# Windowed attention and two expert layers: queries, keys and values laid out as the products read them, value product turned round

## The chip, the cores and the metric

One core of one Trainium2 chip. The metric is the time on the device in microseconds, lower is better; the median of the runs shown is 935.2 us.

## The reference

Three layers stand behind each other, all in float32. First an attention of 4 batches x 8 heads x 768 positions x 64 numbers: each chunk of 32 queries sees 8 memory rows and a window of keys from 16 before the chunk to 8 after it, 64 columns in all.

```python
for c in range(nc):
    q_c = q[:, :, c_start:c_end]
    k_full = np.concatenate([mem_k, k[:, :, l_start:r_end]], axis=2)
    v_full = np.concatenate([mem_v, v[:, :, l_start:r_end]], axis=2)
    scores = scale * np.matmul(q_c, k_full.transpose(0, 1, 3, 2))
    a = np.exp(scores - np.max(scores, axis=-1, keepdims=True))
    a = a / (np.sum(a, axis=-1, keepdims=True) + 1e-09)
    out[:, :, c_start:c_end] = np.matmul(a, v_full)
```

Then `h = x @ w_in`, `g = h * cos(h)`, `g @ w_out` over 3072 rows (512 to 2048 to 512), and then eight experts (512 to 1024 to 512, relu), to which a router sends the rows whose skip score is positive, each with its gate.

## The kernel before, in words

A tile is 128 positions of one batch with all 8 heads; there are 24. Three tiles make a block of 384 rows; there are eight blocks, 0 to 7. PE does the products, ACT and DVE empty the accumulators, SP issues the loads, POOL fills constants and stores gates. The order on each engine is written out by hand and fixed; semaphores tie them.

**Middle layer.** For each of 16 rounds f of a block PE does `up(f)` (L758: 12 matmuls with 384 columns into one of two banks h_ps) and `down(f - 2)` (L774: 9 matmuls with 512 columns into three banks y_ps). Weights and rows are split in a high and a low float32r part, three matmuls per product. ACT takes h_ps out twice (L953, L954), makes the high part of g (L963) and the cosine as a sine (L977); DVE makes the fraction (L1190, L1192), g (L1185) and its low part (L1196). In round 1 ACT also takes the three y banks of the block before (L985, after the sine).

**Sites.** Between these products lie 32 sites a block: site 2f stands on PE behind `up(f)`, site 2f + 1 behind `down`. On ACT site 2f comes after h_ps is taken out, on DVE after g, and site 2f + 1 at the end of the round. ATTENTION (L39) puts the steps for the tiles of the next block on sites that start at 0, 10 and 20. ROUTER (L44) puts the router of the block before on others: x1 (transposes of the output rows, L737) at 4, 7 and 24, logits (L747) at 5, 8 and 25. On one site, steps run in the order of their names. PROLOGUE (L48) does the three tiles of block 0 ahead of everything; block 0 has no router, but splits weights (`in_high`, `in_low`, `out_high`, `out_low`) at the ends of its rounds. Block 7 has no attention.

**One tile of attention before.** SP loads 128 query rows, 4 windows of key rows, and 8 pieces of value windows (L410 to L447), in a batch's first tile also 12 pieces of memory rows; a row of a head is 64 numbers, 256 bytes. PE turns q (L667) and both halves of k (L676) with 4 transposes each, DVE copies q out (L1078), ACT k (L921). `scores` (L690) is 32 small products, 64 instructions: 64 rows of the array, 32 weight columns, 64 moving columns; the output row group is the chunk, and the two row halves of the array are the two heads of a pair, one half after the other. DVE finds the maximum and subtracts it (L1092, L1097), ACT takes the exponential (L926), DVE sums and forms the reciprocal (L1102 to L1106). PE turns the probabilities (L700), ACT copies them (L930), and `values` (L718) is again 32 products with 32 weight columns (probabilities) and 64 moving ones (values), into two banks, queries on partitions. DVE multiplies by the reciprocal (L1113), PE turns the result (L727), and ACT and DVE write its high and low part (L936, L1119), as `up` reads it. All transposes in blocks share one bank, `turn`; a semaphore counts its uses (L64).

Behind the blocks come a sort of the rows by expert and up to 20 slots of 256 rows through an expert each (L859).

Of the kernel before, what the change touches and what calls it, by code (L numbers as in the profile page):

```python
# [25 lines left out]
ALU = mybir.AluOpType  # L26
# [3 lines left out]
P = 128  # L30
CHUNK, LEFT, RIGHT = 32, 16, 8
# [16 lines left out]
PROLOGUE = [("q", 0), ("k0", 0), ("k1", 0), ("scores", 0), ("exp", 0), ("sum", 0), ("probs", 0), ("values", 0),  # L48
            ("q", 1), ("k0", 1), ("k1", 1), ("x", 0), ("w_in", 0), ("scores", 1), ("exp", 1), ("q", 2),
            ("k0", 2), ("k1", 2), ("sum", 1), ("probs", 1), ("w_in", 1), ("values", 1), ("scores", 2), ("x", 1),  # L50
            ("exp", 2), ("sum", 2), ("probs", 2), ("w_in", 2), ("values", 2), ("x", 2)]
SPLIT_FIRST = 3
T_STEPS = ("q", "k0", "k1", "probs", "x", "x1", "logits")
# [17 lines left out]
def program(nc, q, k, v, mem_k, mem_v, w_in, w_out, w_skip, w_gate, w1, w2, out, x_mid):  # L71
    NB, NH, S, HD = q.shape
    NMEM = mem_k.shape[2]
# [24 lines left out]
    with ctx:  # L98
# [37 lines left out]
        q_sb = sb("q_sb", [P, D])  # L136
        k_sb = sb("k_sb", [P, 2, D])
        v_sb = sb("v_sb", [P, CPT, HP * HD])
        qT = sb("qT", [P, HP, P])
        kT = sb("kT", [P, 2, HP, P])  # L140
        probs = sb("probs", [P, HP, 2, WIN])
        probsT = sb("probsT", [P, HP, P])
        x_sb = sb("x_sb", [P, HP, 2, HD])
# [18 lines left out]
        def pre(name, shape):  # L162
            size = 4 * shape[1] * shape[2] * shape[3]
            t = sb(name, shape, offset=at_pre[0])
            at_pre[0] += size
            return t

        q_pre = pre("q_pre", [P, 2, 1, D])
        k_pre = pre("k_pre", [P, 2, 2, D])
# [73 lines left out]
        first_full = {step: sem(f"first_full_{step}") for step in ("q", "k0", "k1", "probs", "x")}  # L243
        first_free = {step: sem(f"first_free_{step}") for step in ("q", "k0", "k1", "probs", "x")}
        pre_qk_ld = [sem(f"pre_qk_ld{n}") for n in range(2)]
        pre_v_ld = [sem(f"pre_v_ld{n}") for n in range(2)]
        memory_done = sem("memory_done")
# [6 lines left out]
        rsum_done = sem("rsum_done")  # L254
        v_full = sem("v_full")
        v_free = sem("v_free")
# [73 lines left out]
        first_bank = {"q": y_ps[:, 0, :], "k0": y_ps[:, 1, :], "k1": y_ps[:, 2, :], "probs": h_ps[:, 0, :], "x": h_ps[:, 1, :]}  # L330


# [6 lines left out]
        def bank(B, step):  # L339
            return first_bank[step] if is_first(B) else turn[:, 0, :]  # L340

        def filled(B, step):
            return first_full[step] if is_first(B) else t_full

        def freed(B, step):
            return first_free[step] if is_first(B) else t_free

        def wait_filled(eng, B, step, j):

            if is_first(B):  # L350
                eng.wait_ge(first_full[step], j + 1)
            else:
                eng.wait_ge(t_full, use(B, step, j) + 1)

        def wait_filled_before(eng, B, step, j):

            if is_first(B):
                wait(eng, first_full[step], j)
            elif j:
                eng.wait_ge(t_full, use(B, step, j - 1) + 1)  # L360
            else:
                wait_filled(eng, B - 1, step, BT - 1)

        def wait_freed(eng, B, step, j):

            if is_first(B):
                eng.wait_ge(first_free[step], j + 1)
            else:
                eng.wait_ge(t_free, use(B, step, j) + 1)

        def tile_of(B, j):

            return BT * (B + 1) + j

# [30 lines left out]
        def _(sp):  # L405
            def heads(array, b, par, lo, hi):

                picked = slice(0, NH) if par is None else slice(par, NH, 2)
                return array[bass.ds(b, 1), picked, lo:hi, :].rearrange("b h p d -> p (b h) d")

            def load_q(to, b, t, ld):
                sp.dma_start(to.rearrange("p (h d) -> p h d", d=HD), heads(q, b, None, t * P, (t + 1) * P)).then_inc(ld, 16)

            def load_k(to, b, t, ld):
                for c in range(CPT):
                    first = t * P + c * CHUNK - LEFT
                    lo, hi = max(first, 0), min(first + CTX, S)
                    r0 = (c % 2) * WIN + NMEM + lo - first
                    sp.dma_start(to[r0:r0 + hi - lo, c // 2, :].rearrange("p (h d) -> p h d", d=HD),  # L419
                                 heads(k, b, None, lo, hi)).then_inc(ld, 16)  # L420

            def load_v_windows(to, b, t, par, ld):
                for c in range(CPT):
                    first = t * P + c * CHUNK - LEFT
# [24 lines left out]
            def load_pre(n):  # L449
# [3 lines left out]
                for par in range(2):  # L453
                    load_v_windows(v_pre[:, n, :, :], 0, n + 1, par, pre_v_ld[n])
# [940 lines left out]
```

## Time and profile before

| what | value |
|---|---|
| median of 3 runs | 935.2 us (934.59 to 935.61) |
| span of the profiled execution | 933.5 us, 21710 instructions |
| mean granted clock of TensorE | 0.964 |
| DMA packets, and those under 512 bytes | 146219, 120580 |
| chain that ended last | PE 85%, DVE 4%, ACT 3% |
| first up product | 49.56 us |

The span goes from the first to the last instruction of the profiled execution; the time of a run is taken around it. "Busy" of PE counts matmuls with modelled ends, so rows in a timeline overlap: what a group takes is read from its start to the start of the next. "PEclk" or clock is the share of 2.4 GHz granted to TensorE.

### The profile page before, as it was taken

What the parts mean: (1) busy time and instruction counts of PE and PEld (TensorE: products, weight loads), DVE (VectorE), ACT (ScalarE), POOL (GpSimd) and SP (SyncE); (2) the same over time, 40 slices, a digit from 0 to 9 for tenths busy, and PEclk for the clock granted to TensorE, in tenths of its full rate; (3) what the DMA queues carried; (4) which work ended last, traced back from release to release, by engine and by line L of the source; (5) the groups of instructions that cost most, each with busy time, mean ns of one, the idle gap of its engine ahead of it and who ended that gap; (6) DMA issues with size and microseconds to landing.
All of it is one profiled execution on the core that took longest, in us unless ns stands there. A gap on an engine that the chain in (4) does not pass through costs nothing.

```text
span 933.5 us, 21710 instructions
## 1 busy us (share of the span) xinstructions
PE 863.6 (93%) x8306; PEld 766.7 (82%) x8307; DVE 542.4 (58%) x1054; ACT 495.5 (53%) x857; POOL 60.0 (6%) x67
## 2 busy tenths in 40 slices
PE   4489999999999999999999999999993698999995
PEld 3478898888888888789888888888982587999994
DVE  2457766565556555555655555555457576666664
ACT  1366666566457556555665565564453154444442
POOL 4000000000000000000000000000002212111110
PEclk9589999999999999999999999999997599999998
DMA  7962214214221422321232223201007347656653
GB/s 152 265 183 51 53 22 120 52 39 113 52 53 23 119 43 43 84 75 37 56 100 52 52 49 93 51 2 68 1 1 248 112 156 265 224 211 214 217 192 111
DMA packets 146219, 94.59 MB, mean 101 GB/s; under 512 B 120580, under 2 KB 120580, under 8 KB 146120
## 3 DMA queue, kind: packets, MB, share of 16 engines
q1 hardware_dynamic: 143144, 87.21, 32.8%
q0 software_dynamic: 2976, 6.05, 1.8%
q8 instruction: 63, 1.03, 0.5%
q14 instruction: 36, 0.29, 0.1%
HBM read 79.33 MB, written 16.79 MB: 103 GB/s over the span
## 4 chain that ended last, share of the span: by engine, by line
PE 85%; DVE 4%; ACT 3%; issue 2%; SPq 2%; DMA 2%; POOL 1%; POOLq 0%; DVEq 0%; ACTq 0%
PE h_ps L769 29%; PE y_ps L783 27%; PE y_ps L884 8%; PE h_ps L869 8%; PE s_ps L690 2%; PE s_ps L718 2%; PE turn L676 2%; DMA xg<-x_mid,idx_from 2%; PE turn L727 1%; PE turn L737 1%; PE turn L667 1%; PE turn L700 1%; SPq L427 1%; SPq L419 1%; PE turn L747 1%
## 5 line engine op out<-in xcount | busy, mean ns | idle before, releaser
L769 PE MATMUL h_ps<-xT_hi,in_hi 128*128 128x384 f32 x512 | 180.9, 353 | 2.1 <-DVE xT_lo L1119 1.4
L769 PE MATMUL h_ps<-xT_lo,in_hi 128*128 128x384 f32 x512 | 172.7, 337 | 1.2 <-issue 1.2
L769 PE MATMUL h_ps<-xT_hi,in_lo 128*128 128x384 f32 x512 | 173.4, 339 | 0.0
L783 PE MATMUL y_ps<-out_hi,g_hi 128*128 128x512 f32 x384 | 159.5, 415 | 1.8 <-DVE g_lo L1196 1.8
L953 ACT ACTIVATE hs<-h_ps 128x384 f32<-128x384 f32 x128 | 62.6, 489 | 180.8 <-PE h_ps L769 179.2
L783 PE MATMUL y_ps<-out_hi,g_lo 128*128 128x512 f32 x384 | 151.1, 393 | 0.0
L783 PE MATMUL y_ps<-out_lo,g_hi 128*128 128x512 f32 x384 | 150.1, 391 | 0.0
L1190 DVE TENSOR_SCALAR whole<-us 128x384 f32<-128x384 f32 x128 | 47.0, 367 | 96.2 <-ACT us L954 95.6
L769 PEld LDWEIGHTS h_ps<-xT_hi,in_hi 128*128 128x128 f32 x512 | 96.7, 189 | 7.0 <-DVE xT_lo L1119 1.8
L977 ACT ACTIVATE us<-us 128x384 f32<-128x384 f32 x128 | 67.3, 526 | 65.4 <-DVE us L1192 61.3
L769 PEld LDWEIGHTS h_ps<-xT_lo,in_hi 128*128 128x128 f32 x512 | 96.9, 189 | 1.8
L769 PEld LDWEIGHTS h_ps<-xT_hi,in_lo 128*128 128x128 f32 x512 | 96.6, 189 | 1.3 <-issue 1.3
L1196 DVE TENSOR_TENSOR g_lo<-hs,g_hi 128x384 fp32r<-128x384 f32 x128 | 71.0, 554 | 28.3 <-ACT g_hi L963 28.3
L783 PEld LDWEIGHTS y_ps<-out_hi,g_lo 128*128 128x128 f32 x384 | 72.0, 188 | 16.5
L783 PEld LDWEIGHTS y_ps<-out_hi,g_hi 128*128 128x128 f32 x384 | 72.2, 188 | 14.9 <-DVE g_lo L1196 2.2
L783 PEld LDWEIGHTS y_ps<-out_lo,g_hi 128*128 128x128 f32 x384 | 72.5, 189 | 11.4
L1185 DVE TENSOR_TENSOR hs<-hs,us 128x384 f32<-128x384 f32 x128 | 71.0, 554 | 12.2 <-ACT us L977 4.3
L869 PE MATMUL h_ps<-xgT_hi,w_hi 128*128 128x256 f32 x256 | 74.0, 289 | 3.0 <-PEq L898 1.6
L1192 DVE TENSOR_TENSOR us<-us,whole 128x384 f32<-128x384 f32 x128 | 71.5, 559 | 4.4
L869 PE MATMUL h_ps<-xgT_lo,w_hi 128*128 128x256 f32 x256 | 73.6, 287 | 0.0
L869 PE MATMUL h_ps<-xgT_hi,w_lo 128*128 128x256 f32 x256 | 73.5, 287 | 0.0
L963 ACT ACTIVATE g_hi<-hs 128x384 fp32r<-128x384 f32 x128 | 67.4, 526 | 7.4 <-DVE hs L1185 7.4
(168 smaller groups left out, 1367.9 us busy)
## 6 DMA issues: line engine op xcount, KB each, us to landing
raw<-w SPq DMA_DIRECT2D x72, 512.0 KB, 5.5
k_sb<-k SPq DMA_DIRECT2D x80, 112.0 KB
v_sb<-v SPq DMA_DIRECT2D x160, 56.0 KB
x_mid<-x SPq DMA_DIRECT2D x24, 256.0 KB, 4.4
out<-x SPq DMA_DIRECT2D x24, 256.0 KB, 5.3
q_sb<-q SPq DMA_DIRECT2D x22, 256.0 KB
in_raw<-w_in SPq DMA_DIRECT2D x4, 1024.0 KB, 5.4
out_raw<-w_out SPq DMA_DIRECT2D x4, 1024.0 KB, 9.7
```

The lines of the kernel that those rows point to most:

```text
L676: last = pe.transpose(to[:, hp * P:(hp + 1) * P], rows[:, hp * P:(hp + 1) * P], ident[:, :])
L769: last = pe.matmul(h_ps[:, f % 2, 0:BN], w[:, dc, f * P:(f + 1) * P], x[:, half, dc, :], start=(n == 0), stop=(n == 3 * DC - 1))
L783: last = pe.matmul(y_ps[:, j, :], g[:, f % RING, j * P:(j + 1) * P], w[:, f, :], start=(f == 0 and n == 0), stop=(f == FT - 1 and n == 2))
L869: last = pe.matmul(h_ps[:, g % 2, (f % 2) * SLOT:(f % 2 + 1) * SLOT], w[:, dc, f * P:(f + 1) * P], x[:, dc, :], start=(n == 0), stop=(n == ...
L884: last = pe.matmul(y_ps[:, a, :], g[:, f, a * P:(a + 1) * P], w[:, f, :], start=(f == 0 and n == 0), stop=(f == EFT - 1 and n == 2))
L953: act.activation(hs[:, f % 2, :], h_ps[:, f % 2, 0:BN], ACT.Copy)
L963: act.activation(g_hi[:, f % RING, :], hs[:, f % 2, :], ACT.Copy).then_inc(ghi_done, 1)
L977: act.activation(us[:, f % 2, :], us[:, f % 2, :], ACT.Sin, scale=TWO_PI).then_inc(cos_done, 1)
L1185: dve.tensor_tensor(hs[:, f % 2, :], hs[:, f % 2, :], us[:, f % 2, :], ALU.mult).then_inc(g_done, 1)
L1190: dve.tensor_scalar(whole[:, :], us[:, f % 2, :], ROUND, ROUND, ALU.add, ALU.subtract).then_inc(whole_done, 1)
L1192: dve.tensor_tensor(us[:, f % 2, :], us[:, f % 2, :], whole[:, :], ALU.subtract).then_inc(frac_done, 1)
L1196: dve.tensor_tensor(g_lo[:, f % RING, :], hs[:, f % 2, :], g_hi[:, f % RING, :].bitcast(F32), ALU.subtract).then_inc(glo_done, 1)
```

## The change

The host lays out q, k and v before the launch. `qk` has per tile a block of 128 partitions (two heads of a pair x 64 numbers) with 4 x 128 columns of queries and 4 x 4 x 64 columns of key windows, memory and zeros included; `v` has per tile 128 partitions (two heads x 64 window rows). So a tile is three loads, with 2, 4 and 4 KB per partition. The transposes of q and k and their copies go. The value product takes the values as weights (64 columns) and the probabilities as moving columns (32), and its result comes out as `up` reads it, in one bank; so the probabilities are divided by their sum before they are turned, and the transposes of the result go. The steps get other sites, `probs` a second buffer, the prologue another order.

```diff
 for _j, _b in enumerate((0, 10, 20)):
-    ATTENTION += [(_b, "q", _j), (_b + 1, "k0", _j), (_b + 2, "k1", _j), (_b + 3, "scores", _j),
-                  (_b + 4, "exp", _j), (_b + 5, "sum", _j), (_b + 6, "probs", _j),
-                  (_b + 8, "values", _j), (_b + 9, "x", _j)]
+    ATTENTION += [(_b + 1, "scores", _j), (_b + 2, "exp", _j), (_b + 3, "sum", _j), (_b + 5, "probs", _j),
+                  (_b + 7, "values", _j), (_b + 8, "x", _j)]
...
+PROLOGUE = [("scores", 0), ("scores", 1), ("exp", 0), ("sum", 0), ("exp", 1), ("probs", 0), ("values", 0),
+            ("sum", 1), ("x", 0), ("scores", 2), ("exp", 2), ("probs", 1), ("values", 1), ("w_in", 0), ("sum", 2),
+            ("x", 1), ("probs", 2), ("values", 2), ("w_in", 1), ("x", 2), ("w_in", 2)]
...
+        def probs_bank(B):
+            return h_ps[:, 0, :] if is_first(B) else turn[:, 0, :]
+
+        def x_bank(B, j):
+            return y_ps[:, j, :] if is_first(B) else s_ps[:, 0, :]
...
+            def load_qk(tile, to_q, to_k, ld):
+                sp.dma_start(to_q, qk[bass.ds(tile, 1), :, 0:HP * P].rearrange("a p n -> (a p) n")).then_inc(ld, 16)
+                sp.dma_start(to_k, qk[bass.ds(tile, 1), :, HP * P:].rearrange("a p n -> (a p) n")).then_inc(ld, 16)
...
-            sp.wait_ge(ready, 2)
-            load_qk(0, 0)
+            load_qk(0, flat(q_sb), flat(k_sb), qk_ld)
+            load_v(0, flat(v_sb), v_ld)
+            load_qk(1, flat(q_pre[:, 0]), flat(k_pre[:, 0]), pre_qk_ld[0])
+            load_v(1, flat(v_pre[:, 0]), pre_v_ld[0])
             load_in(0)
...
+                        if following:
+                            sp.wait_ge(s_full, T + 1)
+                            load_qk(T + 1, flat(q_sb), flat(k_sb), qk_ld)
...
+                        if following:
+                            sp.wait_ge(v_full, T + 1)
+                            load_v(T + 1, flat(v_sb), v_ld)
...
-            pool.memset(k_sb[:, :, :], 0.0).then_inc(ready, 1)
-            pool.memset(v_sb[:, :, :], 0.0).then_inc(ready, 1)
             pool.memset(ident[:, :], 0.0).then_inc(ready, 1)
...
+                    wait(pe, s_free, T)
+                    if not is_first(B):
+                        pe.wait_ge(x_free, T)
                     carry(pe)
+                    queries = q_pre[:, j - 1, :, :] if ahead else q_sb[:, :, :]
+                    windows = k_pre[:, j - 1, :, :, :] if ahead else k_sb[:, :, :, :]
                     for hp in range(HP):
+                        for par in range(2):
+                            rows = slice(par * WIN, (par + 1) * WIN)
                             for c in range(CPT):
                                 last = pe.matmul(
                                     s_ps[c * CHUNK:(c + 1) * CHUNK, par, hp * WIN:(hp + 1) * WIN],
-                                    qT[rows, hp, c * CHUNK:(c + 1) * CHUNK],
-                                    kT[rows, c // 2, hp, (c % 2) * WIN:(c % 2 + 1) * WIN],
+                                    queries[rows, hp, c * CHUNK:(c + 1) * CHUNK],
+                                    windows[rows, hp, c, :],
                                     start=True, stop=True)
                     last.then_inc(s_full, 1)
                 elif step == "probs":
...
+                    pe.wait_ge(norm_done, T + 1)
...
+                    for hp in range(HP):
+                        for c in range(CPT):
+                            for par in range(2):
+                                rows = slice(par * WIN, (par + 1) * WIN)
+                                first = hp * P + c * CHUNK
                                 last = pe.matmul(
-                                    s_ps[c * CHUNK:(c + 1) * CHUNK, par, hp * HD:(hp + 1) * HD],
-                                    probsT[rows, hp, c * CHUNK:(c + 1) * CHUNK],
-                                    windows[rows, c, hp * HD:(hp + 1) * HD], start=True, stop=True)
+                                    to[par * HD:(par + 1) * HD, first:first + CHUNK],
+                                    windows[rows, c, hp * HD:(hp + 1) * HD],
+                                    probsT[rows, hp, c * CHUNK:(c + 1) * CHUNK], start=True, stop=True)
                     last.then_inc(v_full, 1)
...
-                if step in ("k0", "k1"):
-                    wait_filled(act, B, step, j)
-                    wait(act, s_full, T)
-                    act.activation(kT[:, int(step[1]), :, :].rearrange("p h k -> p (h k)"), bank(B, step),
-                                   ACT.Copy).then_inc(freed(B, step), 1)
...
                 elif step == "sum":
...
+                    dve.wait_ge(sum_done, 3 * T + 3)
+                    dve.tensor_tensor(pr, pr, row_sum[:, :, :].unsqueeze(3).to_broadcast([P, HP, 2, WIN]),
+                                      ALU.mult).then_inc(norm_done, 1)
-                elif step == "values":
-                    dve.wait_ge(v_full, T + 1)
-                    dve.wait_ge(rsum_done, T + 1)
...
-                    dve.tensor_tensor(x_sb[:, :, :, :].rearrange("p h a d -> p a h d"),
...
+    keys = windows_of(k, mem_k).transpose(0, 3, 2, 6, 1, 4, 5).reshape(tiles, P, -1)
+    values = windows_of(v, mem_v).transpose(0, 3, 2, 5, 4, 1, 6).reshape(tiles, P, -1)
```

## Rows read from the trace of the kernel before

**Rows 1.** The page: busy time, share and instructions of each engine

```profile
PE 863.6 (93%) x8306; PEld 766.7 (82%) x8307; DVE 542.4 (58%) x1054; ACT 495.5 (53%) x857; POOL 60.0 (6%) x67
```

**Rows 2.** Groups of instructions by line: shapes, count | busy us, mean ns | idle before

```profile
L676 PE MATMUL turn<-ident,k_sb 128*128 128x128 f32 x168 | 25.2, 273 | 0.8 <-DVE qT L1078 0.8
...
L1092 DVE TENSOR_REDUCE row_max<-s_ps 128x8 f32<-128x512 f32 x24 | 16.6, 691 | 15.2 <-PE s_ps L690 15.0
...
L926 ACT ACTIVATE probs<-probs 128x512 f32<-128x512 f32 x24 | 15.1, 631 | 6.5 <-DVE probs L1097 6.2
```

**Rows 3.** Timeline of PE in block 0: start us, us, engine, line, instruction, count

```profile
71.44 0.99 PE L718 MATMUL s_ps<-v_sb,probsT 64*32 64x64 f32 x64
72.36 0.50 PE L783 MATMUL y_ps<-out_hi,g_hi 128*128 128x512 f32 x1
```

**Rows 4.** Chain of waits in block 0: start us, us, engine, result, line, count

```profile
127.15 0.44 PE turn L727 x4
...
129.68 2.08 PE y_ps L783 x9
131.76 2.11 PE h_ps L769 x12
```

**Rows 5.** Timeline of PE in the prologue

```profile
9.04 1.09 PE L667 MATMUL y_ps<-ident,q_sb 128*128 128x128 f32 x4 [9.04 <-DMA k_sb<-mem_k]
9.92 1.91 PE L676 MATMUL y_ps<-ident,k_sb 128*128 128x128 f32 x8
12.77 1.53 PE L690 MATMUL s_ps<-kT,qT 64*32 64x64 f32 x64 [0.93 <-ACT kT L921]
...
31.15 1.12 PE L667 MATMUL y_ps<-ident,q_pre 128*128 128x128 f32 x4 [6.38 <-DMA k_pre<-k]
...
49.56 0.69 PE L769 MATMUL h_ps<-xT_hi,in_hi 128*128 128x384 f32 x1 [1.41 <-DVE xT_lo L1119]
```

**Rows 6.** Timeline of PE in block 2, after its second up product

```profile
221.66 0.60 PE L676 MATMUL turn<-ident,k_sb 128*128 128x128 f32 x4
...
227.38 0.60 PE L737 MATMUL turn<-ident,x 128*128 128x128 f32 x4
...
229.99 0.44 PE L747 MATMUL turn<-wr,x1T 128*32 128x9 f32 x32
230.36 0.44 PE L769 MATMUL h_ps<-xT_hi,in_hi 128*128 128x384 f32 x1
```

**Rows 7.** Timeline of SP's DMA queue, first issue

```profile
2.78 0.45 SPq L412 DMA_DIRECT2D q_sb<-q  x1
```

**Rows 8.** Stretches: us, busy us of PE, PEld, DVE, ACT, POOL; clock, DMA share, GB/s

```profile
36.00:38.00 2.00, 1.14 (x59) 0.89 (x50) 1.57 (x2) 0.40 (x1) 0.00 (x0) 0.50 1.05 406
5.00:10.00 5.00, 0.96 (x5) 0.99 (x6) 0.00 (x0) 0.00 (x0) 0.95 (x1) 1.00 0.86 223
...
775.00:778.00 3.00, 3.00 (x10) 2.35 (x9) 2.52 (x4) 2.90 (x4) 0.00 (x0) 0.59 0.83 304
```

**Rows 9.** Timeline of ACT in block 2

```profile
224.28 1.58 ACT L985 ACTIVATE x<-y_ps 128x512 f32<-128x512 f32 x3
227.58 0.49 ACT L953 ACTIVATE hs<-h_ps 128x384 f32<-128x384 f32 x1 [1.73 <-PE h_ps L769]
...
230.30 0.51 ACT L963 ACTIVATE g_hi<-hs 128x384 fp32r<-128x384 f32 x1
...
232.12 0.53 ACT L977 ACTIVATE us<-us 128x384 f32<-128x384 f32 x1
```

**Rows 10.** Timeline of DVE in block 2

```profile
232.31 0.20 DVE L1106 RECIPROCAL row_sum<-row_sum 128x8 f32<-128x8 f32 x1
```

**Rows 11.** Waits: engine, line <- releaser: us in total, times, longest us

```profile
PE turn L854 <- DMA xg<-x_mid,idx_from: 9.7, 2, 7.5
...
PE turn L727 <- DVE x_sb L1113: 1.2, 2, 0.6
```

More of the change, by code:

```diff
@@ L30 @@
 P = 128
+BATCH, HEADS, SEQ, HEAD_DIM, MEMORY = 4, 8, 768, 64, 8
 CHUNK, LEFT, RIGHT = 32, 16, 8
@@ L162, in pre @@
         def pre(name, shape):
-            size = 4 * shape[1] * shape[2] * shape[3]
+            size = 4
+            for n in shape[1:]:
+                size *= n
             t = sb(name, shape, offset=at_pre[0])
@@ L405, in _ @@
         def _(sp):
[L406 to L420, printed above, removed]
@@ L649, in turn_is_free @@
             def turn_is_free(B, step, j):
[L650 to L653 removed]
+                wait(pe, t_free, use(B, step, j))
             def attend(B, half, step, j):
@@ L754, in site @@
                         route(B, step, j)
-                    else:
+                    elif step in ("scores", "probs", "values"):
                         attend(B, half, step, j)
@@ L1008, in _ @@
                     in_high(j)
-                else:
+                elif step in ("exp", "probs", "x"):
                     attend(-1, 1, step, j)
@@ L1074, in attend @@
                 t = (BT + j) if half == 0 else j
-                if step == "q":
-                    wait_filled(dve, B, step, j)
-                    wait(dve, s_full, T)
-                    dve.tensor_copy(qT[:, :, :].rearrange("p h n -> p (h n)"), bank(B, step)).then_inc(freed(B, step), 1)
-                elif step == "scores":
+                if step == "scores":
                     dve.wait_ge(s_full, T + 1)
@@ L1179, in site @@
                         route(B, step, j)
-                    elif step in ("q", "scores", "sum", "values", "x"):
+                    elif step in ("scores", "sum", "x"):
                         attend(B, half, step, j)
@@ L1217, in _ @@
                     in_low(j)
-                else:
+                elif step in ("scores", "sum", "x"):
                     attend(-1, 1, step, j)
-            dve.wait_ge(ready, 5)
+            dve.wait_ge(ready, 3)
             blocks(dve, run)
@@ L1358, with windows_of @@
 LOOK = 6
-def qk_loads(B, half, j):
-    if half == 1:
-        return 9 if isinstance(B, int) and B == -1 else 17 * (B + 1) + 5 * (j + 1) + 4 - 10
-    return 17 * B + 5 * (3 + j + 1) + 4 - 10
-def v_loads(B, half, j):
-    if half == 1:
-        return 16 if isinstance(B, int) and B == -1 else 28 * (B + 1) + 8 * (j + 1) + 8 - 16
-    return 28 * B + 8 * (3 + j + 1) + 8 - 16
+def windows_of(given, memory):
+    import numpy as np
+    b, h, s, d = given.shape
+    padded = np.zeros((b, h, LEFT + s + RIGHT, d), given.dtype)
+    padded[:, :, LEFT:LEFT + s] = given
+    parts = [np.concatenate([memory, padded[:, :, c:c + LEFT + CHUNK + RIGHT]], axis=2) for c in range(0, s, CHUNK)]
+    cpt = P // CHUNK
+    return np.stack(parts, axis=2).reshape(b, h // 2, 2, s // P, cpt, memory.shape[2] + LEFT + CHUNK + RIGHT, d)
 def kernel(q, k, v, mem_k, mem_v, moe_w_in, moe_w_out, moe2_w_skip, moe2_w_gate, moe2_w1, moe2_w2):
```

288 lines of the change are left out of this document (96 added, 192 removed).

## The prediction, made before the result was known

> **What bounds the kernel now.** I read the page first, then the chain of waits and the timelines of PE, ACT and DVE in the prologue and in one block with a router, then the waits. PE is busy for 93% of the span of 933.5 us, DVE and ACT for less than 60% [rows 1]; the median of the runs is 935.2, so 1.7 us lie around the span, and I add them at the end. The stages are those of the code. From the first up product at 49.56 [rows 5] PE runs through the eight blocks nearly without a gap, so there every PE microsecond that goes is a microsecond of the span, until something else is late. Before 49.56 PE mostly waits; loads and hand-offs bound that part. The expert part at the end is not touched.
>
> **Price of what goes.** Per tile PE loses four groups of four transposes (q, k0, k1, x). In the chain of waits, which goes from end to end, such a group stands with 0.44 us [rows 4], where the row of the group has 273 ns for a single one, its latency [rows 2]. The k row has 168 instructions, 42 groups for 21 tiles; q and x have 84 each. So 4 x 0.44 = 1.75 per tile, 36.7 us for the 21 tiles inside the blocks. ACT loses two copies and DVE one per tile; both wait often, so this is worth nothing by itself. The multiplication by the reciprocal stays one DVE operation over 512 elements, about 0.69 like the maximum [rows 2], but moves ahead of the transposes of the probabilities.
>
> **Price of the turned value product.** No row shows it. It keeps 64 instructions on PE, now with 64 weight columns and 32 moving ones, on two parts of the array instead of four. The present one takes 0.92 from start to start [rows 3]. Full transposes load 128 columns and move 128: 256 columns at 2.4 GHz are 107 ns, at 1.2 GHz 213; measured are 0.44 / 4 = 110 and (9.92 - 9.04) / 4 = 220 [rows 4, 5], so in this data type load and move add up. The present tiled product has 96 columns each on four parts: 16 x 80 ns = 1.28 us at 1.2 GHz, plus a drain, against 1.53 measured [rows 5]. At 2.4 GHz that would be 0.64 but 0.92 is seen, so a floor sits on the instruction: 32 tiny ones take 0.37, 11.6 ns each [rows 6]. On two parts 96 columns cost 32 x 40 ns = 1.28: +0.36 per tile. Bounds: at the floor, 64 x 11.6 = 0.74 (-0.18), and, if the two parts never run together, 64 x 40 = 2.56 (+1.64). I take +0.36, the sum that fits the transposes at both clocks. The scores keep their shapes but alternate between row halves; eight parts instead of four put them at the floor at best: 0.92 to 0.74, and I take -0.17 (bound: 0). Net per tile: -1.75 + 0.36 - 0.17 = -1.56.
>
> For the value product both row halves now write one bank. The Trainium skill, TensorEngine Tiling (Array Packing), Restrictions and Gotchas, says that different row tiles cannot access the same PSUM bank at once; if the chip kept them apart by waiting, the product would cost the upper bound. The halves write different partitions, so I don't take it; it is a rival below. No run here shows it yet.
>
> **The prologue.** SP's first issue is at 2.78 [rows 7], behind two fills of POOL; without them it is some 2 us earlier. Three loads of 0.26 to 0.5 MB stand in place of 13 or 25 small ones per tile, so the queue stops being the limit (PE waited 9.0 and 6.4 us for its first and third tile [rows 5]). At the 406 GB/s of a stretch with large loads [rows 8] the first 0.8 MB take 2 us; first scores near 5, and no later load is late (at the 223 of 5 to 10 us [rows 8] the third tile comes 3 to 5 us late). From there the order decides: scores(0) 1.5 and DVE's two passes with hand-offs to 8.3; scores(1) and its passes to 11.4; sum and normalisation of tile 0, 1.9, to 13.2; transposes and copy to 15.0; values(0) at the low clock, 1.5 + 1.0, to 17.7; scores(2) and DVE to 20.7; exp 0.63 [rows 2] and copy to 22; values(1) to 24.7; sum(2) behind it to 26.1; transposes and copy to 27.9; values(2) to 30.5; hi and lo parts to 32. Against 49.56: **-17.5**, between -21 (product at the floor) and -10 (slow loads).
>
> **What becomes late.** Steps move to other sites; three places look too close. Time from the end of up(1) of a block, U = 221.66 [rows 6].
> - Exp of tile 0 moves from site 4 to 2, into the round in which ACT also empties the three y banks. In the round that has it now, ACT starts at 227.58 and its sine at 232.12, table loads included [rows 9]. Add 0.53 for the sine, 0.6 for the first y copy (0.53 each in the row of three), 0.3 for hand-offs: x1(0) cannot be transposed before U + 6.0. PE used to come at 5.72 [rows 6] with 2.5 to spare; without k1 and scores between, it comes at 2.08 + 2.11 = 4.2 [rows 4]. **Stall 1.8.**
> - At sites 5 and 25 the probabilities are transposed into `turn` right behind the logits, with no product between: PE waits for DVE's copy of the logits. At site 5 DVE is behind fraction and g_lo, done at U + 9.4 against PE's 8.9: **0.6**.
> - At site 25 DVE comes from the normalisation: reciprocal done 5.13 after its U [rows 10], multiplication to 5.9, then g, the x1 copy to 7.1 (PE's logits want it at 6.75: 0.4), fraction and g_lo (0.4 to 0.7 each), the logits copy to 8.6 against PE's 7.5: **1.6** together.
>
> Together 4.0 per block with router and attention, six blocks. SP's three issues per tile follow s_full and v_full and have ten sites for a load. Tile 1 has norm at U + 5.9 and PE at 6.3, just covered. In block 0 (no router) exp at site 2 delays g_lo(0), so down(0) waits 1.85, less than the stalls of turning tile 3 now, which I count as even; two x waits, 1.2, go [rows 11], and some 1.6 come back at sites 13 to 17, where ACT and DVE also split weights.
>
> **Sum.** Prologue -17.5; block 0 3 x -1.56 - 1.2 + 1.6 = -4.3; blocks 1 to 6 6 x (3 x -1.56 + 4.0) = -4.1. 933.5 - 25.9 + 1.7 = **909**.
>
> **Rivals.**
> - The slots are kinder (15%): if ACT and DVE make up half of those stalls, 12 us go: 897; all, 885. For it: my chain adds up rows of the loaded schedule. Against: the queues are in fixed order.
> - The value product runs at the floor (15%): 21 x (0.74 - 1.28) = -11.3 in the blocks and some 4 in the prologue give 894; at the 0.92 of now, 900.
> - The clock (10%): PE waited 7.5 and 2.2 us for gathered rows [rows 11]; behind the second the clock of 775 to 778 is 0.59, between the two levels of 1.2 and 2.4 GHz [rows 8]. If the 1.8 us stall does so, some 1.7 us more a block: 919.
> - The slower side (12%): the two halves of the value product take turns. +1.28 x 21 in the blocks and +2.5 x 3 on the prologue's chain: 909 + 34 = 943. It decides from 2.4 us a product on: 26 us saved, spread over the 24 tiles, are 1.1 on top of 1.28. For it: nothing alternates row halves now except once per product. Against: four column parts run together [rows 3].
> - My forecast (48%), itself 901 to 919. That the transposes remain on PE in another form is excluded by the diff.
>
> **Numbers.** 885 to 919 hold the first three, the clock reaches a little beyond; leaving out the slower rival and the ends of the first, the range is 889 to 927. A measurement can tell about 0.2%, 2 us, from no change. Faster: all but the slower rival and a mishap of the prologue, 0.86; within 0.2% 0.02; slower 0.12.
>
> **What would show it.** No rows of transposes from q, k or x; first up product near 32; the value product with 64 columns of weights at 1.28 from start to start in the blocks (2.56 would be the slower rival, 0.74 the floor); waits of PE's x1 transposes on ACT's y copy, 6 of 1.8, and of the probabilities' transposes on DVE's logits copy, 6 near 0.6 and 6 near 1.2; the clock at 1.00 in blocks 1 to 6; DVE and ACT below 60% busy. The prediction is wrong if the blocks shorten by much more than 9 us in all, or if the first product starts after 40.

## The result, and the profile after

The changed kernel takes 922.5 us in the median of 4 runs (920.39 to 924.2), beside 935.4 (934.59 to 936.21) for the kernel before on the same chip: ratio 0.985, 95% interval [0.9831, 0.9869]. It is faster by 1.5%, less than 2% but clear of the interval. The time lies inside the predicted range, but only 13 us are saved where 26 were forecast. The profiled execution took 920.39 with a span of 918.7 us.

The page of the changed kernel: busy time of the engines, then the DMA line.

```profile
PE 841.1 (92%) x7922; PEld 745.2 (81%) x7923; DVE 525.8 (57%) x1030; ACT 468.6 (51%) x809; POOL 49.4 (5%) x57
...
DMA packets 40685, 97.38 MB, mean 106 GB/s; under 512 B 5852, under 2 KB 5852, under 8 KB 40608
```

PE has lost 384 matmuls against [rows 1], but only 22.5 us of its busy time; the packets are down from 146219 to 40685. The bound is the same engine. To see where the 14.8 us of span (933.5 - 918.7) went, I cut both spans at the first and the last matmul of `up` in the timeline of PE (the last is at 699.02 before and 685.19 after):

| stretch, us | before | after | forecast |
|---|---|---|---|
| prologue, to the first up | 49.56 | 33.99 | -17.5 |
| blocks, first to last up | 649.5 | 651.2 | -8.4 |
| behind the last up | 234.5 | 233.5 | 0 |

The prologue came nearly as foreseen. The blocks did not shorten at all, although 84 groups of transposes left PE there. The timeline of PE in the blocks of the changed kernel shows why (start us, us, engine, line, instruction, count, idle time before it):

```profile
77.94 2.06 PE L642 MATMUL s_ps<-probsT,v_sb 64*64 64x32 f32 x64
79.93 0.45 PE L686 MATMUL h_ps<-xT_hi,in_hi 128*128 128x384 f32 x1
...
88.51 0.86 PE L606 MATMUL s_ps<-k_sb,q_sb 64*32 64x64 f32 x64
89.30 0.44 PE L686 MATMUL h_ps<-xT_hi,in_hi 128*128 128x384 f32 x1
...
209.77 0.65 PE L654 MATMUL turn<-ident,x 128*128 128x128 f32 x4 [1.53 <-ACT x L898]
212.42 0.44 PE L664 MATMUL turn<-wr,x1T 128*32 128x9 f32 x32
213.24 0.66 PE L621 MATMUL turn<-ident,probs 128*128 128x128 f32 x4 [0.38 <-DVE lg L1040]
...
265.36 0.65 PE L621 MATMUL turn<-ident,probs 128*128 128x128 f32 x4 [1.04 <-DVE lg L1040]
```

The turned value product (L642) takes 79.93 - 77.94 = 1.99 us from its start to the start of what follows, where the old one took 0.92 [rows 3] and 1.28 was forecast. The scores (L606) take 0.79. The three stalls stand where they were foreseen: x1 behind ACT's copies of y (1.53), the probabilities behind DVE's copy of the logits at site 5 (0.38) and at site 25 (1.04). The waits of PE in the same kernel (us in total, times, longest):

```profile
PE turn L654 <- ACT x L898: 9.0, 6, 1.5
PE turn L621 <- DVE lg L1040: 8.2, 12, 1.0
PE s_ps L606 <- DMA k_sb<-qk: 5.2, 1, 5.2
PE y_ps L700 <- DVE g_lo L1100: 4.8, 4, 2.3
PE h_ps L621 <- DVE probs L1019: 3.6, 2, 3.3
PE y_ps L642 <- ACT probsT L843: 3.4, 3, 1.8
PE s_ps L606 <- DMA k_pre<-qk: 2.8, 1, 2.8
```

The prologue, in PE's timeline, is shorter by its loads, and its products are slower:

```profile
5.23 1.17 PE L606 MATMUL s_ps<-k_sb,q_sb 64*32 64x64 f32 x64 [5.23 <-DMA k_sb<-qk]
9.18 1.17 PE L606 MATMUL s_ps<-k_pre,q_pre 64*32 64x64 f32 x64 [2.78 <-DMA k_pre<-qk]
13.62 1.11 PE L621 MATMUL h_ps<-ident,probs 128*128 128x128 f32 x4 [3.27 <-DVE probs L1019]
15.52 3.62 PE L642 MATMUL y_ps<-probsT,v_sb 64*64 64x32 f32 x64 [0.78 <-ACT probsT L843]
...
28.95 3.62 PE L642 MATMUL y_ps<-probsT,v_pre 64*64 64x32 f32 x64 [0.78 <-ACT probsT L843]
33.99 0.69 PE L686 MATMUL h_ps<-xT_hi,in_hi 128*128 128x384 f32 x1 [1.41 <-DVE xT_lo L1023]
```

First scores at 5.23 ("near 5"), values(0) at 15.52 (15.0), first up at 33.99 (32): of the 2 us that are missing, the third values product began 1.05 later than foreseen and takes 3.6 where 2.5 were added.

So two things were open. Why does the product take 1.99: is it the form of the instruction, two row halves that write one bank, or halves that take turns? And what are the stalls worth once they are taken away, since a wait that goes can come back at the next semaphore? Beside the experiments the kernel before measured 936.1 to 937.0 us in the median.

### The profile page after: what moved, and what is told of

It reads as the page before. It is cut to its first block, busy times and chain, and to the rows that moved or that the text cites. A ratio compares the mean times of both kernels' runs of the same rounds, so it can differ in the third digit from the quotient of the medians.

```text
span 918.7 us, 20139 instructions
## 1 busy us (share of the span) xinstructions
PE 841.1 (92%) x7922; PEld 745.2 (81%) x7923; DVE 525.8 (57%) x1030; ACT 468.6 (51%) x809; POOL 49.4 (5%) x57
## 4 chain that ended last, share of the span: by engine, by line
PE 77%; DVE 7%; ACT 7%; issue 4%; DMA 3%; POOL 1%; SPq 0%; ACTq 0%; POOLq 0%; DVEq 0%
PE h_ps L686 26%; PE y_ps L700 24%; PE h_ps L787 8%; PE y_ps L802 7%; PE s_ps L642 5%; ACT L839 2%; DMA xg<-x_mid,idx_from 2%; PE s_ps L606 2%; PE turn L621 1%; ACT L890 1%; PE turn L654 1%; ACT us L867 1%; PE y_ps L642 1%; DMA k_pre<-qk 1%; PE turn L664 1%
## 5 line engine op out<-in xcount | busy, mean ns | idle before, releaser
L700 PE MATMUL y_ps<-out_hi,g_hi 128*128 128x512 f32 x384 | 151.9, 396 | 4.8 <-DVE g_lo L1100 4.8
L890 ACT ACTIVATE us<-us 128x384 f32<-128x384 f32 x128 | 67.2, 525 | 68.8 <-DVE us L1096 68.5
L700 PEld LDWEIGHTS y_ps<-out_hi,g_lo 128*128 128x128 f32 x384 | 72.0, 188 | 15.6
```

The costliest lines, as they stand in the source:

```text
L700: last = pe.matmul(y_ps[:, j, :], g[:, f % RING, j * P:(j + 1) * P], w[:, f, :], start=(f == 0 and n == 0), stop=(f == FT - 1 and n == 2))
L890: act.activation(us[:, f % 2, :], us[:, f % 2, :], ACT.Sin, scale=TWO_PI).then_inc(cos_done, 1)
```

## Experiments on the price of the product

**The old product in the new places.** In the blocks the probabilities are the weights again (32 columns), DVE multiplies the result, and four transposes turn it, at site +9.

```diff
-                  (_b + 7, "values", _j), (_b + 8, "x", _j)]
+                  (_b + 7, "values", _j), (_b + 9, "x", _j)]
...
+                    if not is_first(B):
+                        for hp in range(HP):
+                            for par in range(2):
+                                rows = slice(par * WIN, (par + 1) * WIN)
+                                for c in range(CPT):
+                                    last = pe.matmul(
+                                        s_ps[c * CHUNK:(c + 1) * CHUNK, par, hp * HD:(hp + 1) * HD],
+                                        probsT[rows, hp, c * CHUNK:(c + 1) * CHUNK],
+                                        windows[rows, c, hp * HD:(hp + 1) * HD], start=True, stop=True)
...
+                    for hp in range(HP):
+                        last = pe.transpose(turn[:, 0, hp * P:(hp + 1) * P],
+                                            x_sb[:, hp, :, :].rearrange("p a d -> p (a d)"), ident[:, :])
```

> The changed kernel, but inside the blocks the value product is the one of before (32 weight columns of probabilities, 64 moving columns of values, two banks), with DVE's multiplication behind it and four transposes of the result, which go one site later; q, k and v still come laid out. Theory (the turned product is dearer than what it saves): per tile 1.99 goes and 0.92 + 0.44 comes, -0.63, 21 tiles, -13 us: about 909. Rival (the products hardly matter, the stalls decide): within 3 us of 922.5. Where the two halves now alternate in the old shape too, the product could fall to 0.79 as the scores did: then 906.

Measured: 906.3 us (903.23 to 907.37), ratio to the kernel before 0.9676 [0.9647, 0.9706], so 16 us faster than the changed kernel. PE's timeline, product and turn of its result:

```profile
77.77 0.86 PE L644 MATMUL s_ps<-v_sb,probsT 64*32 64x64 f32 x64
78.55 0.45 PE L709 MATMUL h_ps<-xT_hi,in_hi 128*128 128x384 f32 x1
...
82.83 0.60 PE L664 MATMUL turn<-ident,x_sb 128*128 128x128 f32 x4
83.18 0.42 PE L709 MATMUL h_ps<-xT_hi,in_hi 128*128 128x384 f32 x1
83.44 0.34 PE L709 MATMUL h_ps<-xT_lo,in_hi 128*128 128x384 f32 x1
83.62 0.34 PE L709 MATMUL h_ps<-xT_hi,in_lo 128*128 128x384 f32 x1
```

The product takes 0.79. The four transposes take 0.35 from start to start, and the up matmul behind them 0.26 where the next takes 0.18: together about the 0.44 of [rows 4]. So the old way is 1.23 against 1.99: 21 x 0.76 = 16.0 us, as much as the medians differ. The blocks are 17.5 us shorter (633.7 against 651.2), of which 1.6 are waits for the logits copy that became shorter (8.2 to 6.6). Turning the value product round is the part of the change that lost most time. The loops here change the row half after every four instructions, as the scores of the changed kernel do, and with that the old form is also quicker than in the kernel before (0.92), which did all of one half first.

**The halves in turn.** Only the loop order changes: all products of one row half, then all of the other.

```diff
-for hp in range(HP):
-    for c in range(CPT):
-        for par in range(2):
+for par in range(2):
+    for hp in range(HP):
+        for c in range(CPT):
```

> The changed kernel with the two row halves of the turned product one after the other instead of alternating. Theory A (a weight load waits for the load before it, a move runs beside the next load only on another part of the array): without alternation load and move of one part add up, 64 x 40 ns = 2.56 us a product instead of 1.99, time +12 us. Theory B (the halves hinder each other because they write one bank): nothing is left to hinder, the product is no slower than 1.99 and perhaps 1.3 to 1.6. If the parts never ran together, 1.99 stays.

Measured: 987.6 us in one run, span 985.9.

```profile
63.00 3.71 PE L642 MATMUL s_ps<-probsT,v_sb 64*64 64x32 f32 x64
66.64 0.44 PE L686 MATMUL h_ps<-xT_hi,in_hi 128*128 128x384 f32 x1
```

A product now takes 3.64, 57 ns an instruction, which neither theory had foreseen. So in the changed kernel (31 ns) the two halves do run side by side, at least for the most part; they don't take turns. And one instruction alone is dearer than I had it: 64 weight and 32 moving columns are 96, 40 ns at 2.4 GHz; 57 ns are 137 columns. That is 64 + 64 and some 4 ns more, as though the 32 moving columns were counted as 64.

The products alone don't make the run that slow. Its clock was lower too; these are stretches (us, busy us of PE, clock, DMA share, GB/s):

```profile
50.00:650.00 600.00, 580.12 (x5371) 0.96 0.19 61
116.00:119.40 3.40, 3.40 (x64) 1.00 0.00 0
119.60:122.80 3.20, 3.20 (x11) 0.50 0.48 164
```

A product runs at the full clock from 115.90 to 119.54; behind it the clock is 0.50 for 3.4 us, and an up matmul takes 0.32 from start to start instead of 0.18. Between 50 and 650 us there are twelve such falls. Eleven begin within 1 us of the end of a value product, one behind a wait of 2.06. At half the clock PE needs twice the time, so a mean of 0.96 over 600 us is 24 us lost; the changed kernel has 1.00 there.

**A bank for each half.** The second half writes another bank; ACT and DVE then read the result in two pieces.

```diff
+                                half_to = s_ps[:, par, :] if not is_first(B) else to
                                 last = pe.matmul(
-                                    to[par * HD:(par + 1) * HD, first:first + CHUNK],
+                                    half_to[par * HD:(par + 1) * HD, first:first + CHUNK],
```

> The changed kernel, but inside the blocks the second half of the turned product goes to a bank of its own; ACT and DVE then read the result in two pieces of 64 partitions (about 0.6 and 0.7 us more per tile, beside PE's work). Theory A (weight loads): the product stays at 1.99. Theory B (one bank): it falls to 1.28 or less. By the rule on row tiles and one PSUM bank in the Trainium skill, TensorEngine Tiling (Array Packing), Restrictions and Gotchas, it would fall as well.

Measured: 939.4 us in one run, 17 us above the changed kernel. PE's timeline and its waits:

```profile
79.00 2.06 PE L643 MATMUL s_ps<-probsT,v_sb 64*64 64x32 f32 x64
80.98 0.45 PE L687 MATMUL h_ps<-xT_hi,in_hi 128*128 128x384 f32 x1
```

```profile
PE y_ps L701 <- DVE g_lo L1116: 16.8, 25, 2.3
```

The product is unchanged at 1.98, so the shared bank costs nothing here, and the rule that I had weighed in the prediction (the Trainium skill, TensorEngine Tiling (Array Packing), Restrictions and Gotchas) does not show as a delay. The extra time is a cost of the experiment: ACT and DVE have one more operation per tile each (689 ns on DVE), and g_lo is late 25 times instead of 4. These waits are 12.0 of the 19.0 us of span that it adds; the rest was not traced.

**64 moving columns instead of 32.** Each instruction moves the columns of two chunks, with the same weights and the same count. So the kernel leaves out the right result of the attention; only the product's own duration is read.

```diff
-                                first = hp * P + c * CHUNK
+                                first = hp * P + min(c, CPT - 2) * CHUNK
+                                at_q = min(c, CPT - 2) * CHUNK
                                 last = pe.matmul(
-                                    to[par * HD:(par + 1) * HD, first:first + CHUNK],
+                                    to[par * HD:(par + 1) * HD, first:first + 2 * CHUNK],
                                     windows[rows, c, hp * HD:(hp + 1) * HD],
-                                    probsT[rows, hp, c * CHUNK:(c + 1) * CHUNK], start=True, stop=True)
+                                    probsT[rows, hp, at_q:at_q + 2 * CHUNK], start=True, stop=True)
```

> The changed kernel with 64 instead of 32 moving columns in each of the 64 instructions of the turned product (it streams the neighbouring chunk as well, so part of the attention's result is not what the reference asks for, and the rows go to the experts otherwise; only the product's own duration is read). Theory (a move counts as at least some 64 columns: the two halves in turn cost 57 ns an instruction, which is 64 + 64 columns at 2.4 GHz and 4 ns, and 52.5 ns each, alternating at 1.2 GHz, is half of 128 columns): the product stays near 1.99. Rival (load 64 and move 32 add up, with a fixed 17 ns on top): 32 more columns are 13.3 ns more an instruction on two parts, 1.99 + 0.43 = 2.4.

Measured: 922.99 us in one run.

```profile
78.89 2.08 PE L643 MATMUL s_ps<-probsT,v_sb 64*64 64x64 f32 x64
80.91 0.45 PE L687 MATMUL h_ps<-xT_hi,in_hi 128*128 128x384 f32 x1
```

2.02 against 1.99: twice the moving columns cost next to nothing. So with the halves alternating a move of 32 columns costs what one of 64 does. This is what the Trainium skill says under TensorEngine Tiling (Array Packing), Instruction Overhead: a matmul with few free columns takes as long as one with about 60. The two runs (1.99 and 2.02) agree with it. That the weight load of 64 columns comes on top is argued from the 57 ns of the halves in turn; 64 moving columns were not tried in that order.

**Weights of 32 columns.** The turned product in halves of a head: 128 instructions, each with 32 weight columns, on four parts of the array instead of two (the "eight" in the expectation is a slip: each row half has two column groups).

```diff
-                            for par in range(2):
...
-                                    to[par * HD:(par + 1) * HD, first:first + CHUNK],
-                                    windows[rows, c, hp * HD:(hp + 1) * HD],
...
+                            for part in range(2):
+                                for par in range(2):
...
+                                    lo = par * HD + part * 32
+                                    last = pe.matmul(
+                                        to[lo:lo + 32, first:first + CHUNK],
+                                        windows[rows, c, hp * HD + part * 32:hp * HD + (part + 1) * 32],
```

> The changed kernel with each weight load of the turned product split in two of 32 columns, so 128 instructions on eight parts of the array instead of 64 on two. Theory (a part pays for its load and for at least 64 moving columns; with eight parts only the issue of instructions is left, 12.3 ns each in the scores): 128 x 12.3 = 1.57 instead of 1.99, 21 x 0.42 = 9 us less. Rival (the number of moves counts, whatever the parts): 128 instead of 64 moves make it 3 us or more.

Measured: 903.6 us in one run, span 901.9.

```profile
75.53 1.29 PE L644 MATMUL s_ps<-probsT,v_sb 64*32 64x32 f32 x128
76.75 0.44 PE L688 MATMUL h_ps<-xT_hi,in_hi 128*128 128x384 f32 x1
```

Twice as many instructions take 1.22 instead of 1.99, cheaper than the 1.57 expected. An instruction of 32 weight and 64 counted moving columns is 96 columns, 40 ns; on four parts that gives 10, and 9.5 ns are measured. For the turned product, then, the price in both forms is near columns over parts in use (31 ns measured against 27 for the 64-wide one), and 64-wide weights leave two parts where there could be four. This is no rule for every small product: the scores have 96 columns an instruction too, and take 14.4 ns (0.92 / 64) with four parts at a time. The blocks are 16.0 us shorter (635.2 against 651.2), and 21 x 0.77 = 16.2.

**The scores with their halves in turn.** The scores' loop as in the old order, all else as changed.

```diff
-for hp in range(HP):
-    for par in range(2):
+for par in range(2):
+    for hp in range(HP):
```

> The changed kernel with the scores' two row halves one after the other, as before the change. Theory (the fall of the scores from 0.92 to 0.79 is the alternation): 0.92 again, 21 x 0.13 = 3 us more. Rival (it is the operands, which now lie in other buffers): 0.79 stays.

Measured: 928.7 us in one run; the timeline of PE:

```profile
65.11 0.99 PE L606 MATMUL s_ps<-k_sb,q_sb 64*32 64x64 f32 x64
66.04 0.44 PE L686 MATMUL h_ps<-xT_hi,in_hi 128*128 128x384 f32 x1
```

0.93 again, as before the change, so it is the alternation, here after every four instructions, that made 0.79 of 0.92. Its span of 927.1 is 8.4 above the changed kernel's: 3.9 in the blocks, of which 21 x 0.14 = 2.9 are this, 1.3 in the prologue, and 3.2 behind the last up, which the edit does not touch; those I put down to the scatter of single runs.

## Experiments on the stalls

**Router sites alone.** The x1 and logits steps move to sites where ACT and DVE should be through.

```diff
-ROUTER = [(4, "x1", 0), (5, "logits", 0), (7, "x1", 1), (8, "logits", 1), (24, "x1", 2),
-          (25, "logits", 2), (26, "route", 0), (27, "rexp", 0), (28, "gate", 0)]
+ROUTER = [(8, "x1", 0), (9, "logits", 0), (10, "x1", 1), (12, "logits", 1), (18, "x1", 2),
+          (20, "logits", 2), (26, "route", 0), (27, "rexp", 0), (28, "gate", 0)]
```

> The changed kernel with one list altered: x1 and logits of the router move from sites 4/5, 7/8 and 24/25 to 8/9, 10/12 and 18/20. Theory (stalls): the 17.2 us in which PE waits for ACT's y copy (9.0) and for DVE's logits copy (8.2) are real and go; 922.5 falls to about 905, with both waits near zero. Rival (the queues only pass the lateness on): ACT and DVE are as late at another place, so PE waits elsewhere and less than 5 us are gained, 918 or more.

Measured: 914.95 us (911.68 to 917.49), ratio 0.9753 [0.9719, 0.9787]. The waits of PE:

```profile
PE y_ps L700 <- ACT x L898: 8.9, 6, 1.5
PE y_ps L700 <- DVE g_lo L1100: 4.2, 3, 2.1
```

The logits waits are gone (8.2 us), the x1 wait is not: it stands now before the down product, which needs the same banks emptied (`down` with f = 0 waits for y_free). Six waits of 1.5 before, six of 1.5 after. The cause is not where x1 is turned but that ACT is late with the y copies. The profiled execution gains 2.9 us of span (915.8), the medians 7.5. The changed kernel's profiled execution is the fastest of its four runs and this one the slowest of its own. The blocks, from first to last up, are 5.5 us shorter (645.7 against 651.2), although in this run the clock stood at 0.50 from 46.5 to 49.7, behind a wait of 2.08 of down(0) for g_lo, which costs some 1.7. So the gain is 5 to 8 us, near the waits for the logits alone.

**The attention sites moved.** The turned product stays; the exponential goes behind the round in which ACT empties the y banks, and all that follows with it.

```diff
-    ATTENTION += [(_b + 1, "scores", _j), (_b + 2, "exp", _j), (_b + 3, "sum", _j), (_b + 5, "probs", _j),
-                  (_b + 7, "values", _j), (_b + 8, "x", _j)]
+    ATTENTION += [(_b + (2 if _j else 1), "scores", _j), (_b + 4, "exp", _j), (_b + 5, "sum", _j), (_b + 7, "probs", _j),
+                  (_b + 9, "values", _j), (_b + 10, "x", _j)]
...
+ROUTER = [(4, "x1", 0), (5, "logits", 0), (8, "x1", 1), (10, "logits", 1), (13, "x1", 2),
+          (15, "logits", 2), (26, "route", 0), (27, "rexp", 0), (28, "gate", 0)]
```

> The changed kernel with the steps on other sites: exp of the first tile two sites later, behind the round in which ACT empties the y banks, and no x1 or probabilities right behind logits (scores 1, 12, 22; exp 4, 14, 24; sum, probs, values, x at 5, 7, 9, 10 and on; x1 4, 8, 13, logits 5, 10, 15). Theory (the waits come from exp in the round of the y copies: moving the router alone only handed the 9.0 us from x1 on to down(0), which wants the y banks empty as well): both waits go, 17 us, 922.5 to about 905, ratio to before 0.966. Rival (ACT and DVE have too much work for the shorter blocks): the waits come back elsewhere and it stays above 912, as when the router's steps alone were moved.

Measured: 913.55 us (909.61 to 914.81), ratio 0.9733 [0.9696, 0.9771]. The waits of PE:

```profile
PE y_ps L700 <- DVE g_lo L1100: 7.5, 12, 1.8
...
PE h_ps L686 <- issue: 2.4, 1, 2.4
...
PE h_ps L686 <- DVE xT_lo L1023: 1.9, 4, 1.4
```

Both waits, 17.2 us, are gone, and the span is only 5.9 shorter (918.7 to 912.8; by the medians 8.9); the time stays above 912, as the rival had it. The rows name 2.7 more for g_lo, 1.2 more of issue (1.2 in the changed kernel at the same place), 0.5 more for xT_lo, and 1.6 in the expert part, which is untouched. Behind the 2.4 us of issue the clock fell:

```profile
364.00:367.00 3.00, 3.00 (x10) 0.50 0.00 0
```

With up matmuls at 0.32 instead of 0.18 this is some 1.7 us more. The last 3 to 4 were not traced further.

**Only the layout, with the old sites.** The old product in the blocks, as in the first experiment above, and the sites of the kernel before for what is left of the steps; the router as it was. This is the change without its turned product and without its moved sites.

```diff
-    ATTENTION += [(_b + 1, "scores", _j), (_b + 2, "exp", _j), (_b + 3, "sum", _j), (_b + 5, "probs", _j),
-                  (_b + 7, "values", _j), (_b + 8, "x", _j)]
+    ATTENTION += [(_b + 3, "scores", _j), (_b + 4, "exp", _j), (_b + 5, "sum", _j), (_b + 6, "probs", _j),
+                  (_b + 8, "values", _j), (_b + 9, "x", _j)]
```

> Only the queries, keys and values laid out by the host, and what follows from that (no turns of them, no copies, the prologue of the changed kernel, the normalization on VectorE after the exp), with the value product as it was and the attention sites of the kernel before: scores 3, exp 4, sum 5, probs 6, values 8, x 9, and the router sites of before. Theory (what the changed kernel loses inside its blocks is two things, the product's own price and its sites one to two places earlier, where ACT is still held for the down product's banks): against the run with the old product in the new places, 906.3, the waits behind the x1 turns (9.0) and behind the logits (6.6) go, and nothing takes their place: 889, between 886 and 895. Rival (there is always a wait of about this size once PE runs ahead of ACT and VectorE, and it only moves to the down product's g_lo): 900 or more, with over 6 us of waits of the down products for g_lo.

Measured: 888.8 us (885.73 to 890.57), ratio to the kernel before 0.9471 [0.9418, 0.9525]. The waits of PE in it:

```profile
PE y_ps L723 <- DVE g_lo L1141: 3.4, 2, 1.8
PE h_ps L709 <- issue: 2.2, 2, 1.6
...
PE turn L664 <- DVE x_sb L1058: 1.9, 2, 1.1
```

Neither the x1 nor the logits wait is among them, and nothing of their size has come instead. Against the old product in the new places the span went from 901.6 to 888.3, by 13.3 us; the blocks alone went from 633.7 to 617.2, by 16.4 us for 15.6 us of waits, while the prologue (0.7) and the part behind the last up (2.4), which the edit does not touch, came out longer. The new sites were the second part of the change that lost time.

**The turned product in 32-column weights, near the old sites.**

```diff
+    ATTENTION += [(_b + 3, "scores", _j), (_b + 4, "exp", _j), (_b + 5, "sum", _j), (_b + 7, "probs", _j),
+                  (_b + 9, "values", _j), (_b + 10, "x", _j)]
+ROUTER = [(4, "x1", 0), (5, "logits", 0), (8, "x1", 1), (10, "logits", 1), (24, "x1", 2),
           (25, "logits", 2), (26, "route", 0), (27, "rexp", 0), (28, "gate", 0)]
```

> The changed kernel with its turned product in weights of 32 columns and the attention sites 3, 4, 5, 7, 9, 10 (the router's second tile at 8 and 10, the rest as it was). Theory (price of the product and sites are separate and add up): the run with 32-column weights alone gave 903.6 with 9.0 of waits behind the x1 turns and 8.2 behind the logits; without these, and with about 1 to 3 back in waits for g_lo, 889, between 885 and 895; and beside the run with the old product at these sites it is within 4 us, since that has the four transposes (1.75 less the rest of the product's 1.2 against 0.79: 1.3 a tile, 27 in all, so it should if anything be slower by more). Rival (the waits come back at the down products, as in the run with the exps moved, where half returned): 895 to 900.

Measured: 888.1 us (886.99 to 888.67), ratio to the kernel before 0.947 [0.9421, 0.9519], on the same chip as the run above. The page, and the waits of PE:

```profile
PE 824.1 (93%) x9458; PEld 727.9 (82%) x9459; DVE 526.1 (59%) x1030; ACT 469.4 (53%) x809; POOL 50.0 (6%) x57
```

```profile
PE y_ps L702 <- DVE g_lo L1102: 4.3, 6, 1.8
...
PE h_ps L688 <- DVE xT_lo L1025: 1.9, 4, 1.4
...
PE h_ps L688 <- issue: 1.5, 1, 1.5
```

The 889 is met and the two gains add up: 0.77 a tile from the product, and 15.1 us of span (901.9 to 886.8), 15.7 in the blocks, from the sites. The bracket in my expectation that this version should win by 27 us more was a slip: 1.75 is the price of all four groups of transposes of a tile, and only one of them, 0.44, belongs to the old value product. Rightly worked out both ways cost the same, 0.79 + 0.44 = 1.23 and 1.22. The medians say so as well (888.8 and 888.1), but by two differences that offset each other: the prologue with 32-column weights is 2.6 us shorter (first up at 32.32 against 34.94), its blocks 2.2 longer (619.5 against 617.2). Both beat the kernel before and the changed one.

## Why the prediction was half right

The range of 889 to 927 held the 922.5 by its width. The product alone moves the forecast from 909 to 924, near the upper end, and kinder stalls took some of it back.

**The bound, the removed transposes and the clock: right.** PE stayed the bound (92% busy) and its clock stayed at full speed, as the row of the stretch from 40 to 680 us shows (us, busy us of PE, clock, DMA share, GB/s):

```profile
40.00:680.00 640.00, 618.23 (x6080) 1.00 0.18 60
```

That a group of transposes is worth 0.44 and not its latency of 4 x 273 ns holds: the version with the layout alone loses three groups a tile and 0.13 on each of two products, 21 x (1.31 + 0.13 + 0.13) = 33.0, and its stretch of blocks is 617.2 us (34.94 to 652.18) against 649.5, that is 32.3 less.

**The value product: the step that failed.** "On two parts 96 columns cost 32 x 40 ns = 1.28" was fitted to full transposes at both clocks and to the old tiled product, none of which moves fewer than 64 columns in that sum. The runs put about 64 + 64 columns in its place (57 ns alone, 31 with both halves side by side; 2.02 with 64 columns really moved). The term is +1.07 a tile, not +0.36: 0.71 x 21 = 14.9 us lost against the forecast. My upper bound of 2.56 held it, but only as the price of another mechanism, that the halves take turns, which is refuted. I had taken the floor from 32 tiny instructions with nine moving columns, 11.6 ns each on four parts [rows 6]. Read per part that is 46 ns, for 32 + 9 columns that would be 17: the row that should have told me. The same row was in my prediction as the floor of any instruction, and 9.5 ns measured with 32-column weights shows that it is none.

**The scores: right.** -0.17 forecast, -0.13 measured, and alternation is the cause.

**The stalls: right in place, a little large.** The x1 wait was forecast with 6 x 1.8 and measured at 6 x 1.5; the logits with 0.6 and 1.2 and measured at 0.38 and 1.04 (the 0.4 for the x1 copy at site 25 did not appear). Together 17.2 us where 24 were in the sum. What I left out is that they were the price of a choice: taking the sites back returned 13 to 15 us of span, 16 in the blocks (both pairs of runs), and nothing took their place.

**Block 0.** The wait of down(0) for g_lo is there, 2.3 us with 1.85 foreseen.

**The prologue: right but for the same term.** -17.5 forecast, -15.6 measured. The profile's clock column says 1.00 there, as for the stretch from 5 to 10 in [rows 8], but up matmuls take 0.32 until 37.0, as at a granted 0.50, and 0.18 after it; so I take the stretch as one of the 1.2 GHz level, as the prediction did. A product takes 19.07 - 15.52 = 3.55 us, 55 ns an instruction, where 2.5 us a product were counted: 128 columns at 1.2 GHz are 107 ns, over two parts 53.

**The sum for the blocks.** Forecast -8.4. Product +14.9, scores +0.9, stalls -6.8 give +0.6 against +1.7 measured; about 1 us stays unassigned.

**The rivals.** Kinder slots gave 6.8 us of the 12 that this case asked. The product at the floor was wrong; the opposite held. The halves in turn were built, and give 987.6, not 943. Against the changed kernel its span is 67.2 longer: 21 x (3.64 - 1.99) = 34.7 are the products in the blocks, 8.9 the prologue (first up at 42.88), and the 23.6 that are left agree with the 24 us that the clock took, which fell behind half of its products. That the slow products brought it down is read from the order in time, and no run varied it. The clock rival: in the changed kernel a fall behind the 1.5 us waits did not happen (1.00 from 50 to 650 us), nor behind the 2.3 us of block 0; with other sites it fell once in each of two runs, behind waits of 2.1 and 2.4, and cost the 1.7 that the rival had named.

## What to carry to other kernels

Before turning a product round to save transposes, estimate it from columns per part of the array in both forms: weights plus moving columns, the latter taken as at least 64 here, divided by the parts that work at once. The scores show that the estimate can be too low, so time the product itself as well. Change the row half often, and split wide weights where that fills more parts. The transposes saved were worth 0.44 us a tile; the turned form cost 1.07 more than the old product as it was written, and 0.30 more with 32-column weights (0.43 against the old form with its halves alternating). When steps drop out of a hand-written order, leave the others where they were first, measure, and move them only after that: here the moved sites alone cost 13 to 16 us on the engines that the page shows as half idle. And where a wait is taken away, look for who else needs the same buffer emptied, as the down product did.

## What the runs showed that I had not expected

- In float32 a small product with 64 weight columns costs nearly the same with 32 and with 64 moving columns (1.99 and 2.02 us for 64 instructions on two parts).
- 128 instructions with 32-column weights on four parts take 1.22 us, 64 with 64-column weights on two parts 1.99: twice the instructions, 0.6 of the time.
- Changing the row half after every four instructions, instead of once, takes the same 64 small instructions from 0.92 to 0.79; for the turned product, with a change at every instruction instead of once, it is 1.99 against 3.64. What sets the 0.79 is open: 12.3 ns an instruction is more than the 9.5 seen with 32 moving columns, so it is not a floor on the instruction.
- Two row halves writing different partitions of one bank cost nothing against two banks (1.99 and 1.98).
- With the row halves in turn the clock fell to 0.50 at the end of eleven of the 21 products in the blocks, though PE had no wait in them; all falls together cost 24 us.
